# Keys and queries of an attention layer turned by VectorE in squares of 32 instead of by TensorE

## The chip, the cores and the metric

One core of one Trainium2 chip runs one fused kernel. The metric is the device time of one execution in microseconds. TensorE (PE) multiplies matrices and can turn a 128x128 tile by a product with the identity; VectorE (DVE), ScalarE (ACT) and GpSimd (POOL) work elementwise; SyncE (SP) issues all the DMAs, on one queue that 16 DMA engines serve.

## What is computed

Attention with 4 sink keys and a sliding window of 128, then two feed-forward layers on its output. In float32 throughout:

```python
scores = q @ k.T / sqrt(64)                  # q, k, v: (2, 8, 768, 64)
keep = is_sink | ((rel >= 0) & (rel < 128))  # 4 sinks, window of 128
a = softmax(where(keep, scores, -1e9))
x = (a @ v), heads side by side              # (1536, 512)
p = domain_probs / sum(domain_probs)
x = sum_e p[:, e] * (relu(x @ w1[e]) @ w2[e])     # 4 experts, 1024 wide
h = x @ w_in; out = (h * cos(h)) @ w_out          # 2048 wide
```

## The kernel before, in words

The 1536 tokens are T = 12 tiles of 128; tiles 0 to 5 are the first sequence, 6 to 11 the second. The attention runs in ROUNDS = 27 rounds, numbered i from 0; tile t has rounds 2t and 2t+1, with four heads in each. Every engine has its own list of instructions in program order, and semaphores tie the lists together. An engine that waits holds up all that is behind in its list.

In a round PE makes the scores of two pairs of heads (`scores`, L1406), turns the weights of the round before (`turn_weights`, L1417), turns the next keys in an odd round and the next queries in an even one (`turn_keys`, L1349, and `turn_queries`, L1368: four turns of 128x128 into `turn_bank`), and multiplies the weights of three rounds ago with the values (`weigh_values`, L1441; the sinks' part is L1455, the turn of the sinks' weights and sums L1382). Round i, odd, turns the keys of tile (i+3)/2; round i, even, the queries of tile i/2+1. The scores of a pair wait until the masks of the pair two before it are done, since they share two pairs of banks.

DVE merges and masks the scores (`merge`, L1042, `mask_head`, L1058), then copies the turned keys out of PSUM (`copy_keys`, L1069), in an odd round; the turned queries are copied by ACT (L796), but for tiles 7, 8 and 9 by DVE (`copy_queries`, L1075). It then does the sinks and the inverses of the sums (L1082 to L1099), and in some rounds sums of weights (L1121, rounds 8 and 10) or of tokens (L1129, rounds 18 to 23) for the first feed-forward block, and the low halves of its tokens (`tokens_lo`, L1136). ACT takes the exponentials (L779) and copies the turned weights out (L787). POOL cuts the turned weights to the window (`part_weights`, L595 and L598), and in every even round from 6 on it multiplies a tile of the output by its inverse sums (`normalise`, L651), which come back from memory by DMA (`store_inverse`, L428, and `load_norm`, L436).

SP issues in a written order. Keys (L410), queries (L416) and values (L422) of a tile are loads of 256 KB in pieces of 256 bytes, 1024 of them. After the weights w1 (L443), the values of tile 2 and the probabilities (L506), a loop over t issues `load_norm(t-3)`, `load_keys(t+3)`, `store_inverse(t-2)`, `load_queries(t+3)` and `load_values(t)`.

After round 24 PE goes over to the feed-forward blocks, which fill the rest of the time; their first products are put between the last rounds of attention.

## Time and profile before

| | |
|---|---|
| runs, median (lowest to highest) | 835.33 us (834.03 to 837.50) |
| profiled execution, whole | 837.64 us |
| its span | 835.9 us |
| PE busy | 831.0 us, 99% of the span |
| VectorE busy | 455.7 us, 55% |
| ScalarE busy | 458.0 us, 55% |
| GpSimd busy | 551.7 us, 66% |
| DMA queue of SP | 100976 packets, 69.58 MB, 28.5% of 16 engines |
| attention, from the first product to the last values | about 3 to 95 us |

The profile is one execution. Its page has busy times, the span cut into 40 slices, the DMA queues, and the chain of work that ended last. The trace behind it gives each instruction's start, and for an idle time what ended it. The granted clock is 1.00 in every stretch.

### The profile page before, as it was taken

To read this page: it belongs to the slowest core of one execution; us is meant where nothing else is said; L and a number is where in the kernel's file an instruction comes from. 1 tells how busy PE (TensorE), PEld (TensorE's weight loads), DVE (VectorE), ACT (ScalarE), POOL (GpSimd) and SP (SyncE) were. 2 spreads that over 40 slices of the span, in tenths; PEclk is the share of its full clock that TensorE was granted. 3 is DMA by queue.
4 is the path that set the end of the run, shared out by engine and by line. 5 is a ranking of instruction groups with operands and counts; after the bars stand their busy time and mean duration, and the time that the engine had idled before them with its cause. 6 is when DMAs were issued, how large, how long until landed. Compare 5 with 4: busy or idle time off the path is not lost.

```text
span 835.9 us, 13778 instructions
## 1 busy us (share of the span) xinstructions
PE 831.0 (99%) x4564; PEld 743.6 (89%) x4564; DVE 455.7 (55%) x947; ACT 458.0 (55%) x985; POOL 551.7 (66%) x417
## 2 busy tenths in 40 slices
PE   9999999999999999999999999999999999999998
PEld 7777989988988988988988998998998998998997
DVE  4988833523523427633433433338767749756756
ACT  5888734334334435433423523525867869867864
POOL 3777996476476778575475575878384399685450
PEclk9999999999999999999999999999999999999999
DMA  8785231211221220432331131130223430530202
GB/s 184 169 190 147 67 123 51 102 61 44 98 68 44 91 83 19 117 105 53 95 112 50 52 101 51 51 101 30 73 63 76 125 117 0 177 102 18 84 1 76
DMA packets 101045, 70.46 MB, mean 84 GB/s; under 512 B 68368, under 2 KB 74864, under 8 KB 100976
## 3 DMA queue, kind: packets, MB, share of 16 engines
q1 hardware_dynamic: 100976, 69.58, 28.5%
q8 instruction: 39, 0.64, 0.3%
q14 instruction: 30, 0.25, 0.1%
HBM read 62.96 MB, written 3.19 MB: 79 GB/s over the span
## 4 chain that ended last, share of the span: by engine, by line
PE 96%; DVE 1%; issue 1%; ACT 1%; DMA 0%; SPq 0%; ACTq 0%; DVEq 0%
PE scores L1499 11%; PE scores L1503 11%; PE scores L1501 11%; PE scores L1512 10%; PE scores L1514 10%; PE scores L1510 10%; PE bank L1512 5%; PE bank L1514 5%; PE bank L1510 5%; PE bank L1499 3%; PE bank L1501 3%; PE bank L1503 3%; PE scores L1406 2%; PE bank L1441 2%; PE bank L1417 1%
## 5 line engine op out<-in xcount | busy, mean ns | idle before, releaser
L665 POOL TENSOR_TENSOR w_lo<-w_raw,w_hi 128x512 fp32r<-128x512 f32 x96 | 129.8, 1362 | 139.0 <-ACT w_hi L814 139.0
L1499 PE MATMUL scores<-x_hi,w_hi 128*128 128x384 f32 x528 | 177.1, 335 | 0.4 <-DVE x_lo L1136 0.2
L1503 PE MATMUL scores<-x_hi,w_lo 128*128 128x384 f32 x528 | 176.8, 335 | 0.0
L1501 PE MATMUL scores<-x_lo,w_hi 128*128 128x384 f32 x528 | 176.5, 334 | 0.0
L672 POOL TENSOR_TENSOR w_lo<-w_raw,w_hi 128x1024 fp32r<-128x1024 f32 x48 | 116.2, 2431 | 65.4 <-ACT w_hi L824 65.4
L824 ACT ACTIVATE w_hi<-w_raw 128x1024 fp32r<-128x1024 f32 x48 | 50.9, 1060 | 190.2 <-PE scores L1514 188.8
L1514 PE MATMUL scores<-w_hi,h_lo 128*128 128x512 f32 x384 | 149.3, 389 | 0.0
L1512 PE MATMUL scores<-w_lo,h_hi 128*128 128x512 f32 x384 | 149.3, 389 | 0.0
L1510 PE MATMUL scores<-w_hi,h_hi 128*128 128x512 f32 x384 | 149.0, 388 | 0.0
L1240 DVE SCALAR_TENSOR_TENSOR acc<-scores,probs,acc 128x512 f32<-128x512 f32 x56 | 41.8, 749 | 116.5 <-PE scores L1514 116.5
L1499 PEld LDWEIGHTS scores<-x_hi,w_hi 128*128 128x128 f32 x528 | 99.1, 188 | 2.4 <-issue 0.7
L1501 PEld LDWEIGHTS scores<-x_lo,w_hi 128*128 128x128 f32 x528 | 99.1, 188 | 0.9
L1503 PEld LDWEIGHTS scores<-x_hi,w_lo 128*128 128x128 f32 x528 | 99.1, 188 | 0.0
L665 POOL TENSOR_TENSOR w_lo<-w_sum,w_hi 128x768 fp32r<-128x768 f32 x48 | 92.5, 1928 | 0.0
L1514 PEld LDWEIGHTS scores<-w_hi,h_lo 128*128 128x128 f32 x384 | 72.1, 188 | 14.9
L1510 PEld LDWEIGHTS scores<-w_hi,h_hi 128*128 128x128 f32 x384 | 72.1, 188 | 14.1
L1512 PEld LDWEIGHTS scores<-w_lo,h_hi 128*128 128x128 f32 x384 | 72.1, 188 | 14.0
L1512 PE MATMUL bank<-w_lo,h_hi 128*128 128x512 f32 (+1 forms) x196 | 76.0, 388 | 0.0
L1514 PE MATMUL bank<-w_hi,h_lo 128*128 128x512 f32 (+1 forms) x196 | 75.9, 387 | 0.0
L1510 PE MATMUL bank<-w_hi,h_hi 128*128 128x512 f32 (+1 forms) x196 | 75.8, 387 | 0.0
L660 POOL TENSOR_TENSOR w_sum<-w_raw 128x512 f32<-128x512 f32 x46 | 59.5, 1293 | 15.8 <-DMA w_raw<-in_moe_w_in_dram 13.6
L1204 DVE SCALAR_TENSOR_TENSOR h_lo<-scores,h_hi 128x384 fp32r<-128x384 f32 x64 | 35.5, 554 | 44.1 <-ACT h_hi L878 42.6
(140 smaller groups left out, 1548.0 us busy)
## 6 DMA issues: line engine op xcount, KB each, us to landing
w_raw<-in_moe_w_dram SPq DMA_DIRECT2D x30, 1024.0 KB, 5.1
w_raw<-in_moe_w_in_dram SPq DMA_DIRECT2D x8, 1024.0 KB, 5.0
w_raw<-in_moe_w_out_dram SPq DMA_DIRECT2D x8, 1024.0 KB, 5.4
v_nat<-in_v_dram SPq DMA_DIRECT2D x12, 256.0 KB, 4.0
norm<-routing_dram SPq DMA_DIRECT2D x24, 128.0 KB, 3.2
x_t<-t_sum SPq DMA_DIRECT2D x192, 16.0 KB, 1.9
k_nat<-in_k_dram SPq DMA_DIRECT2D x11, 256.0 KB, 3.8
q_nat<-in_q_dram SPq DMA_DIRECT2D x11, 256.0 KB, 3.6
```

The source lines that it names most:

```text
L660: nc.gpsimd.tensor_tensor(*weight_sum(n)).then_inc(w1_summed, 1)
L665: nc.gpsimd.tensor_tensor(w1_slots(w1_lo, h % 2, part), w1_part(h % 2, part), w1_slots(w1_hi, h % 2, part).bitcast(F32), ALU.subtract)\
L672: nc.gpsimd.tensor_tensor(w2_lo[:, i::2], w2_raw[:, i::2], w2_hi[:, i::2].bitcast(F32), ALU.subtract)\
L824: nc.scalar.activation(w2_hi[:, i::2], w2_raw[:, i::2], ACT.Copy).then_inc(w2_hi_ready, 1)
L1204: nc.vector.scalar_tensor_tensor(h_part(h_lo, h % 2, c), c_source(h % 2, c), 0.0, h_part(h_hi, h % 2, c).bitcast(F32), ALU.max, ALU.subtract)\
L1240: kept_one = nc.vector.scalar_tensor_tensor(acc[:, n], down_bank[k][:], probs[:, n, e:e + 1], acc[:, n], ALU.mult, ALU.add)
L1499: nc.tensor.matmul(target[:, 0:HALF], w1_hi[:, i, slot, d], x_hi[:, n - 1, d], start=first and d == 0, stop=False, skip_group_check=True)
L1501: nc.tensor.matmul(target[:, 0:HALF], w1_hi[:, i, slot, d], x_lo[:, n - 1, d], start=False, stop=False, skip_group_check=True)
L1503: last = nc.tensor.matmul(target[:, 0:HALF], w1_lo[:, i, slot, d], x_hi[:, n - 1, d], start=False, stop=d == 1, skip_group_check=True)
L1510: nc.tensor.matmul(target[:, cols], h_hi[:, i, f, toks], w2_hi[:, c, cols], start=i == 0 and f == 0, stop=False, skip_group_check=True)
L1512: nc.tensor.matmul(target[:, cols], h_hi[:, i, f, toks], w2_lo[:, c, cols], start=False, stop=False, skip_group_check=True)
L1514: return nc.tensor.matmul(target[:, cols], h_lo[:, i, f, toks], w2_hi[:, c, cols], start=False, stop=i == 1 and f == 1, skip_group_check=True)
```

## The change

The keys of the second sequence (tiles 6 to 11) and the queries of tiles 7, 8 and 9 no longer pass through PE. SP loads them in pieces of 32 elements (128 bytes), so that each square of 32x32 lands at the place where its turned form belongs, and one `nc.vector.transpose` of 128x512 turns the sixteen squares of a tile in place of the copy out of PSUM. The squares lie in memory that x_hi and x_lo take later. A key load has 24 pieces on each of 32 partitions (768), and there are 16; a query load has 12 on each (384), and there are 16. They are issued in turns t = 1 to 5 of SP's loop: 6, 6 and 4 of keys, then 8 and 8 of queries. `copy_keys` of tile 6 waits for all 16 key loads, the turn of the queries of tile 7 for all 16 of queries. The loads of keys 6 to 11 and of queries 7 to 9 by L410 and L416 go. In DVE's list `sum_tokens(3)` moves from round 23 to behind three `tokens_lo`.

```diff
-QUERIES_BY_DVE = (7, 8, 9)
+SQUARE_QUERIES = (7, 8, 9)
...
+    SQUARE_KEYS = TPB
...
+            def load_squares(dst, src, first, last, part, signal):
+
+                h = part // 2
+                p, r = divmod(h, 2)
+                for f in range(2):
+                    rows = slice((2 * r + f) * 32, (2 * r + f + 1) * 32)
+                    source = src[1, h, (first - TPB) * P:(last - TPB) * P, f * 32:(f + 1) * 32]
+                    sp.dma_start(dst[rows, p, :].rearrange("j (c i) -> j c i", i=32),
+                                 source.rearrange("(c j) i -> j c i", j=32)).then_inc(signal, 16)
...
-                if 5 <= t + 3 < T:
+                if 5 <= t + 3 < SQUARE_KEYS:
                     load_keys(t + 3)
                 if t >= 2:
                     store_inverse(t - 2)
-                if 5 <= t + 3 < T:
+                if 5 <= t + 3 < T and t + 3 not in SQUARE_QUERIES:
                     load_queries(t + 3)
                 if 3 <= t < T:
                     load_values(t)
+                if t in (1, 2, 3):
+                    for part in range(((0, 6, 12, 16)[t - 1]), (0, 6, 12, 16)[t], 2):
+                        load_key_squares(part)
+                elif t in (4, 5):
+                    for part in range(8 * (t - 4), 8 * (t - 3), 2):
+                        load_query_squares(part)
...
             def copy_keys(t):
-                dve.wait_ge(k_turned, t + 1)
+                if t < SQUARE_KEYS:
+                    dve.wait_ge(k_turned, t + 1)
+                else:
+                    dve.wait_ge(k_squares_landed, 16 * 16)
...
+                    n = t - SQUARE_KEYS
+                    nc.vector.transpose(target, k_squares[:, :, n * P:(n + 1) * P]).then_inc(k_ready, 1)
+
+            def turn_queries(t):
+
+                dve.wait_ge(q_squares_landed, 16 * 16)
                 dve.wait_ge(scores_done, PAIRS * (t - 1))
...
+                nc.vector.transpose(q_t[:, t % 2], q_squares[:, :, n * P:(n + 1) * P]).then_inc(q_squares_ready, 1)
...
-                if i in (18, 20, 21, 23):
-                    sum_tokens((18, 20, 21, 23).index(i))
-                if i == 22:
-                    tokens_lo(0, 0)
+                if i in (18, 20, 21):
+                    sum_tokens((18, 20, 21).index(i))
+                if i in (22, 23):
+                    tokens_lo(0, (22, 23).index(i))
                 if i == ND:
-                    tokens_lo(0, 1)
                     tokens_lo(0, 2)
+                    sum_tokens(3)
                     tokens_lo(0, 3)
                     tokens_lo(0, 4)
...
-                if i % 2 == 1 and (i + 3) // 2 < T:
+                if i % 2 == 1 and (i + 3) // 2 < SQUARE_KEYS:
                     turn_keys((i + 3) // 2)
-                elif i >= 2 and i % 2 == 0 and i // 2 + 1 < T:
+                elif i >= 2 and i % 2 == 0 and i // 2 + 1 < T and i // 2 + 1 not in SQUARE_QUERIES:
                     turn_queries(i // 2 + 1)
```

SP's list between the probabilities and the values of tile 4, before:

```order
L506 DMA probs_in<-in_moe_domain_probs_dram 128x12x4
L410 DMA k_nat<-in_k_dram 128x8x64
L428 DMA routing_dram<-inverse 8x128
L416 DMA q_nat<-in_q_dram 128x8x64
L436 DMA norm<-routing_dram 64x4x128 x2
L410 DMA k_nat<-in_k_dram 128x8x64
L428 DMA routing_dram<-inverse 8x128
L416 DMA q_nat<-in_q_dram 128x8x64
L422 DMA v_nat<-in_v_dram 128x8x64
L436 DMA norm<-routing_dram 64x4x128 x2
L410 DMA k_nat<-in_k_dram 128x8x64
```

and now, up to the values of tile 4 (the lines are those of the changed kernel):

```order
L543 DMA probs_in<-in_moe_domain_probs_dram 128x12x4
L445 DMA k_squares<-in_k_dram 32x24x32 x6
L428 DMA k_nat<-in_k_dram 128x8x64
L465 DMA routing_dram<-inverse 8x128
L435 DMA q_nat<-in_q_dram 128x8x64
L445 DMA k_squares<-in_k_dram 32x24x32 x6
L473 DMA norm<-routing_dram 64x4x128 x2
L465 DMA routing_dram<-inverse 8x128
L435 DMA q_nat<-in_q_dram 128x8x64
L459 DMA v_nat<-in_v_dram 128x8x64
L445 DMA k_squares<-in_k_dram 32x24x32 x4
L473 DMA norm<-routing_dram 64x4x128 x2
```

Six square loads stand ahead of the keys of tile 5, and twelve ahead of the first `norm`; the later loads of k_nat are gone.

PE's list in rounds 12 and 13, before:

```order
L1406 MATMUL scores<-k_t,q_t 128x128 x4
L1417 MATMUL bank<-ident,weights 128x128 x4
L1368 MATMUL bank<-ident,q_nat 128x128 x4
L1455 MATMUL bank<-sink_t,v_sink 128x128 x4
L1441 MATMUL bank<-weights_t,v_nat 64x128 x8
L1406 MATMUL scores<-k_t,q_t 128x128 x4
L1417 MATMUL bank<-ident,weights 128x128 x4
L1349 MATMUL bank<-ident,k_nat 128x128 x4
L1382 MATMUL bank<-ident,sink_w 104x128
L1441 MATMUL bank<-weights_t,v_nat 64x128 x8
```

and now:

```order
L1464 MATMUL scores<-k_t,q_t 128x128 x4
L1475 MATMUL bank<-ident,weights 128x128 x4
L1513 MATMUL bank<-sink_t,v_sink 128x128 x4
L1499 MATMUL bank<-weights_t,v_nat 64x128 x8
L1464 MATMUL scores<-k_t,q_t 128x128 x4
L1475 MATMUL bank<-ident,weights 128x128 x4
L1437 MATMUL bank<-ident,sink_w 104x128
L1499 MATMUL bank<-weights_t,v_nat 64x128 x8
```

Four turns are gone from each of the two rounds; nine rounds (9, 11 to 17 and 19) change in this way.

## Rows read from the trace of the kernel before

**Rows 1.** The page: busy PE, and the DMA share in 40 slices of the span

```profile
PE 831.0 (99%) x4564; PEld 743.6 (89%) x4564; DVE 455.7 (55%) x947; ACT 458.0 (55%) x985; POOL 551.7 (66%) x417
DMA  8785231211221220432331131130223430530202
```

**Rows 2.** Busy time by stretch: start:end, length, engines' busy us (instructions), clock, DMA share, GB/s

```profile
20.00:40.00 20.00, 19.95 (x201) 15.33 (x197) 17.78 (x82) 16.30 (x62) 14.24 (x26) 1.00 0.79 181
46.77:75.37 28.60, 28.60 (x290) 22.83 (x292) 23.54 (x113) 25.46 (x93) 21.32 (x35) 1.00 0.67 166
100.00:120.00 20.00, 20.00 (x95) 17.23 (x94) 7.76 (x13) 7.03 (x12) 19.77 (x15) 1.00 0.30 97
```

**Rows 3.** Chain of work that ended last, rounds 13 and 14: start, us, what

```profile
50.48 0.44 PE bank L1349 x4
50.92 0.11 PE bank L1382
...
53.73 0.44 PE bank L1368 x4
```

**Rows 4.** Timeline of round 7: start, us, engine, line, what

```profile
29.12 1.16 PE L1406 MATMUL scores<-k_t,q_t 64*128 64x264 f32 x8
29.89 0.43 DVE L1042 COPY_PREDICATED scores<-in_prev,scores 128x256 f32<-128x256 int32 x1
30.71 0.60 PE L1349 MATMUL bank<-ident,k_nat 128*128 128x128 f32 x4
32.37 0.94 PE L1406 MATMUL scores<-k_t,q_t 64*128 64x264 f32 x6
32.59 0.30 DVE L1099 COPY inverse<-bank 8x128 f32<-8x128 f32 x1
```

**Rows 5.** DVE's copies out of PSUM and turns of squares: ns min/median/max, first and last start

```profile
L1069 DVE COPY k_t<-bank x11: 687/687/691, 9.5 to 70.4; 128x512 f32<-128x512 f32 x11
L1075 DVE COPY q_t<-bank x3: 687/689/691, 47.9 to 60.9; 128x512 f32<-128x512 f32 x3
L1264 DVE STREAM_TRANSPOSE t_sum<-acc x12: 668/686/712, 338.3 to 648.2; 128x512 f32<-128x512 f32 x12
```

**Rows 6.** SP's issues on the timeline; the time is that of issuing

```profile
20.23 0.84 SPq L506 DMA_DIRECT2D probs_in<-in_moe_domain_probs_dram  x1
21.12 4.57 SPq L410 DMA_DIRECT2D k_nat<-in_k_dram  x1
...
28.39 1.35 SPq L436 DMA_DIRECT2D norm<-routing_dram  x2
```

**Rows 7.** The load of keys issued at 21.12 us: from issue to landing

```profile
DMA to landing us min/median/max: 7.1/7.1/7.1
```

**Rows 8.** DMA in 8 to 9.25 us (pieces of 256 bytes)

```profile
DMA packets 1346, 0.34 MB, mean 271 GB/s; under 512 B 1346, under 2 KB 1346, under 8 KB 1346
q1 hardware_dynamic: 1346, 0.34, 124.5%
```

**Rows 9.** DMA in 23.5 to 24 us (mostly the probabilities, pieces of 16 bytes)

```profile
DMA packets 939, 0.07 MB, mean 132 GB/s; under 512 B 933, under 2 KB 933, under 8 KB 937
```

**Rows 10.** DMA in 350 to 358 us (pieces of 128 bytes, sparse)

```profile
q1 hardware_dynamic: 1737, 0.20, 15.6%
```

**Rows 11.** Timeline of rounds 9 to 12, the places that wait for a load or for DVE

```profile
38.13 1.09 PE L1441 MATMUL bank<-weights_t,v_nat 128*64 128x128 f32 x16
38.57 0.69 DVE L1069 COPY k_t<-bank 128x512 f32<-128x512 f32 x1
...
43.75 0.42 DVE L1042 COPY_PREDICATED scores<-in_prev,scores 128x256 f32<-128x256 int32 x1
46.73 0.42 PEld L1417 LDWEIGHTS bank<-ident,weights 128*128 128x128 f32 x4 [0.27 <-ACT weights L779]
```

**Rows 12.** POOL's first product with a norm, and its wait

```profile
32.83 1.27 POOL L651 TENSOR_TENSOR x_t<-x_t,norm 128x512 f32<-128x512 f32 x1 [3.02 <-DMA norm<-routing_dram]
```

**Rows 13.** PE's first instruction of the second product of the feed-forward layer

```profile
87.31 0.44 PE L1499 MATMUL scores<-x_hi,w_hi 128*128 128x384 f32 x1 [0.20 <-DVE x_lo L1136]
```

More of the change, by code:

```diff
@@ L108, in sem @@
             return ctx.enter_context(nc.semaphore(name))
+        early = ExitStack()
+        sb("early_hi", [P, 2, 2, HALF], stack=early)
+        q_squares = sb("q_squares", [P, PAIRS, HALF], stack=early)
+        sb("early_lo", [P, 5, 2, HALF], stack=early)
+        k_squares = sb("k_squares", [P, PAIRS, S], stack=early)
+        early.close()
         x_hi = sb("x_hi", [P, 7, 2, HALF], F32R)
@@ L186, in program @@
         first_landed = [sem("first_keys_landed"), sem("first_queries_landed")]
+        k_squares_landed = sem("k_squares_landed")
+        q_squares_landed = sem("q_squares_landed")
         probs_landed = sem("probs_landed")
@@ L204, in program @@
         q_ready = sem("q_ready")
+        q_squares_ready = sem("q_squares_ready")
         k_sink_kept = sem("k_sink_kept")
@@ L291, in prev_at, with turned_by_pe @@
             return SLOT - own_at(t)
+        def turned_by_pe(t):
+            return sum(n not in SQUARE_QUERIES for n in range(t))
         def heads(src, t):
@@ L414, in load_queries, with load_key_squares, load_query_squares @@
                 if t >= 2:
-                    sp.wait_ge(q_turned, t - 1)
+                    before = max(n for n in range(t) if n % 2 == t % 2 and n not in SQUARE_QUERIES)
+                    sp.wait_ge(q_turned, turned_by_pe(before) + 1)
                 sp.dma_start(q_nat[:, t % 2, :].rearrange("p (h d) -> p h d", h=H), heads(q, t))\
                     .then_inc(q_landed[t % 2], 16)
+            def load_squares(dst, src, first, last, part, signal):
[6 more added lines that the diff above has]
+                                 source.rearrange("(c j) i -> j c i", j=32)).then_inc(signal, 16)
+            def load_key_squares(part):
+                load_squares(k_squares, k, SQUARE_KEYS, T, part, k_squares_landed)
+            def load_query_squares(part):
+                load_squares(q_squares, q, SQUARE_QUERIES[0], SQUARE_QUERIES[-1] + 1, part, q_squares_landed)
             def load_values(t):
@@ L791, in copy_queries @@
             def copy_queries(t):
-                act.wait_ge(q_turned, t + 1)
+                act.wait_ge(q_turned, turned_by_pe(t) + 1)
                 if t >= 2:
@@ L923, in _ @@
                     exp_head(i, 3)
-                if i >= 2 and i % 2 == 0 and i // 2 + 1 < T and i // 2 + 1 not in QUERIES_BY_DVE:
+                if i >= 2 and i % 2 == 0 and i // 2 + 1 < T and i // 2 + 1 not in SQUARE_QUERIES:
                     copy_queries(i // 2 + 1)
@@ L1068, in copy_keys @@
                     dve.wait_ge(k_sink_kept, (t - 3) // TPB + 1)
-                nc.vector.tensor_copy(k_t[:, :, t % 3, 0:P], turn_bank[:].rearrange("p (k s) -> p k s", k=PAIRS))\
-                    .then_inc(k_ready, 1)
-            def copy_queries(t):
-                dve.wait_ge(q_turned, t + 1)
+                target = k_t[:, :, t % 3, 0:P]
+                if t < SQUARE_KEYS:
+                    nc.vector.tensor_copy(target, turn_bank[:].rearrange("p (k s) -> p k s", k=PAIRS))\
+                        .then_inc(k_ready, 1)
+                else:
+                    n = t - SQUARE_KEYS
+                    nc.vector.transpose(target, k_squares[:, :, n * P:(n + 1) * P]).then_inc(k_ready, 1)
+            def turn_queries(t):
+                dve.wait_ge(q_squares_landed, 16 * 16)
                 dve.wait_ge(scores_done, PAIRS * (t - 1))
-                nc.vector.tensor_copy(q_t[:, t % 2], turn_bank[:].rearrange("p (k s) -> p k s", k=PAIRS))\
-                    .then_inc(q_ready, 1)
+                n = t - SQUARE_QUERIES[0]
+                nc.vector.transpose(q_t[:, t % 2], q_squares[:, :, n * P:(n + 1) * P]).then_inc(q_squares_ready, 1)
             def copy_sinks(t):
@@ L1152, in _ @@
                     copy_keys((i + 3) // 2)
-                elif i % 2 == 0 and i // 2 + 1 in QUERIES_BY_DVE:
-                    copy_queries(i // 2 + 1)
+                elif i % 2 == 0 and i // 2 + 1 in SQUARE_QUERIES:
+                    turn_queries(i // 2 + 1)
                 if i % 2 == 0 and 0 <= (i - 2) // 2 < T:
@@ L1360, in turn_queries @@
             def turn_queries(t):
-                pe.wait_ge(q_landed[t % 2], 16 * (t // 2 + 1))
+                pe.wait_ge(q_landed[t % 2], 16 * sum(n % 2 == t % 2 and n not in SQUARE_QUERIES for n in range(t + 1)))
                 if t == 1:
                     pe.wait_ge(first_ready, 2)
+                elif t < SQUARE_KEYS:
+                    pe.wait_ge(k_ready, t)
                 else:
-                    pe.wait_ge(k_ready, t)
+                    pe.wait_ge(q_ready, turned_by_pe(t) - 1)
                 target = out_bank if t == 1 else turn_bank
@@ L1390, in scores @@
                 else:
-                    pe.wait_ge(q_ready, t)
+                    if t in SQUARE_QUERIES:
+                        pe.wait_ge(q_squares_ready, SQUARE_QUERIES.index(t) + 1)
+                    else:
+                        pe.wait_ge(q_ready, turned_by_pe(t))
                     pe.wait_ge(k_ready, t)
```

## The prediction

> **What bounds the kernel now.** I read the page first: PE is busy 99% of the span, while the other three compute engines have a third or more of it free, and the DMA queue is near its full share only in the first slices [rows 1]. Then the stretches: PE has no idle time to speak of in attention, and none later, where DVE does 7.76 us of work in 20 [rows 2]. So a microsecond taken from PE's list in attention moves all that follows it, and so does each microsecond for which PE is made to wait there. DVE is close behind: 17.78 of 20 us in 20 to 40 us. So is the DMA queue, at a share of 0.79 in the same stretch [rows 2]. The change takes from the first and adds to the last, so the question is whether the loads come in time.
>
> **What goes from PE.** In the chain of work four turns of keys take 0.44 us of PE's time, and four turns of queries as much [rows 3]. Nine such steps go: 9 x 0.44 = 3.96 us. Two of them, in rounds 9 and 11, lie where PE waits for others: between round 10 and round 12 DVE carries the sums of weights, round 11's masks start only when those end, and PE's turn of weights in round 12 waits for ACT behind them [rows 11]. Removing PE's work ahead of that wait brings nothing. Seven are left: 7 x 0.44 = 3.1 us.
>
> **Whether DVE can follow.** From round 12's masks to round 21's PE has 28.6 us of work in 28.6 us and DVE 23.54 [rows 2]. Less 3.1, PE still has 25.5, so DVE is not the bound over the whole. It is in single rounds. An odd round such as 7 costs PE 3.25 us (29.12 to 32.37) and DVE 3.0 (29.89 to 32.89) [rows 4]. PE falls to 2.81, DVE stays, and in rounds 17 and 19, where work is dense on both, some 0.2 to 0.3 us each is not gained. I take 2.6 of the 3.1.
>
> **What DVE does instead.** Nine copies out of PSUM of 687 to 689 ns become nine turns of the same 128x512. The kernel already has this turn, out of SBUF: 668 to 712 ns, median 686 [rows 5]. So the exchange costs nothing either way: 9 x 0.03 us at the extremes, 0.2 us up or down. PSUM is left alone and k_t is written as before.
>
> **The move at the end.** Before, PE's second product waits 0.20 us for a `tokens_lo` of DVE that stands behind `sum_tokens(3)` [rows 13]. With the sum moved back that wait goes, a gain of 0.2 us at most 0.3. The sum feeds the last of the seven products, some microseconds later, so its delay is hidden by the products before it.
>
> **What the DMA queue gets.** Key squares: 16 x 768 = 12288 pieces of 128 bytes, query squares 16 x 384 = 6144; the nine loads that go had 9216 of 256 bytes. The bytes are the same, the pieces double, and they come all at once, from 21 to some 45 us. The price of a piece is the open term. Three rows bound it. Pieces of 256 bytes in a full queue: 1346 in 1.25 us, 0.93 ns a piece for the 16 engines together [rows 8]. Pieces of 16 bytes: 939 in 0.5 us, 0.53 ns [rows 9]. Pieces of 128 bytes, but between places on chip and thinly spread: 15.6% of 16 engines for 8 us over 1737 pieces, 11.5 ns of one engine, 0.72 ns for the 16 together [rows 10]. I take 0.72, the row of this size and also the middle of the others. Above 0.93 lies one more bound: counted as engine time, the 256-byte piece takes 124.5% x 16 x 1250 / 1346 = 18.5 ns, or 1.16 ns a piece if pieces stop overlapping [rows 8].
>
> **When the loads come.** Before, SP is held for 4.57 us while it issues the keys of tile 5, to 25.7 us, since the weights and the probabilities are still in the queue; they land at 21.12 + 7.1 = 28.2 us [rows 6, 7]. That is 1.55 us after their own 0.95 us of pieces. Now six square loads (4608 pieces, 3.3 us) stand ahead of them: 31.5 us. PE wants them at 30.71 [rows 4], so it waits 0.8 us.
>
> All key squares: from 25.7 on the queue has 12288 x 0.72 = 8.8 us of squares, four ordinary loads (keys 5, queries 5 and 6, values 3) of 0.95 = 3.8, and the first norm, 256 KB at 271 GB/s = 1.0. That ends at 39.4 and lands at 40.9. DVE wants them for tile 6 in round 9, where it now starts the copy at 38.57 [rows 11]. It stands in the list until 40.9: **2.3 us late** (the 0.8 is inside this). Queued behind it are the sinks, the masks of round 10 and the sums of weights, which leave no idle time, so PE in round 12 is 2.3 us late too.
>
> Beside it: values 3 land at 38.7, PE wants them at 38.13 + 0.8, in time. The first norm lands at 36.8, 4.0 us late. POOL waits for it already (3.02 us, to 32.83) and has the cutting of weights for PE's round 9 behind it [rows 12], about 2.5 us after that start, so 39.3 where PE would come at 38.9: 0.4 us, hidden under the 2.3. Query squares: two norms, two loads of values and 6144 pieces more, 1.0 + 0.95 + 2.2 twice, end at 47.7 and land at 49.3; DVE wants them at 47.9 + 2.3 = 50.2 [rows 5]. In time, with 0.9 us to spare.
>
> **The sum.** + 2.3 (late squares) - 2.6 (turns) - 0.2 (end) = -0.5 us. The span of 835.9 becomes 835.4. The profiled execution took 837.64 in all, 2.3 us more than the median of the runs; I set the change against the median: 835.33 - 0.5 = **834.8 us**.
>
> **Rivals.**
>
> A, the squares come in time. At 0.53 ns a piece the keys of tile 5 land at 30.6 and all key squares at 38.5, just when they are wanted. Then nothing is late: -2.6 - 0.2 = -2.8, **832.5 us**. For it: the 16-byte row. Against: a square is eight times as long. The Trainium skill ("DMA: Bandwidth & Descriptors", section "Why small descriptors are slow (HBM only)") gives a packet a fixed 3 cycles beside one for each 32 bytes; 256 bytes are 11 cycles and 128 are 7. By that rule, as an estimate, the piece costs 0.59 ns, near this rival. The trace agrees only in part: 16-byte pieces should then be four times cheaper than 256-byte ones, and are less than two times.
>
> B, the squares are as dear as whole pieces, and the wait for them replaces the turns. At 1.16 ns the keys of tile 5 land at 33.5, all key squares at 47.2 (8.7 late), the query squares at 58.9 where DVE wants them at 56.6: 11 us late, less 2.8: +8.2, **843.5 us**. It turns slower by over 0.5% once DVE is 7 us late, from about 1.06 ns a piece. For it: the source is memory, read by half rows, and each load writes only 32 partitions. Against: the engines did overlap pieces in every full stretch.
>
> B', the same at 0.93 ns: 4.9 us late for the keys, 5.3 for the queries, +2.5: **837.8 us**, no measurable change.
>
> C, all nine turns count, and the loads are in time: -3.96 - 0.2, **831.1 us**. It needs rounds 9 to 11 to be less tied to DVE than rows 11 say.
>
> D, that PE's turns don't go. The order shows four fewer in each of nine rounds; no chance of its own.
>
> **Chances.** Forecast 0.33, A 0.24, B' 0.19, C 0.10, B 0.14. 0.5% is 4.2 us, about what a measurement of this kernel can tell from no change. Faster by more: only C, 0.10. Slower by more: B, 0.14. Within: 0.76. The range goes from C, 831.0, to a little above B', 838.5, and leaves out B.
>
> **What would show it.** PE's matmuls fall by 36, and rounds 13 to 16 are 0.44 us shorter each. The key load for tile 5 lands near 31.5 us, and PE waits up to 1 us in round 7. DVE's first turn of k_squares has an idle time ahead of it that ends by DMA at about 41 us; idle there under 0.5 us is A, over 5 is B. The turn takes 0.69 us. The wait of PE's second product is gone. What would make all of it wrong: SP held at another point of its list, so that a norm or a load of values comes later than the squares do, or one engine of the 16 with a longer queue than the others, since a load lands with its last.

## The result, and the profile after the change

The kernel before took 834.68 us in these runs (median, 833.92 to 837.5), the changed one **843.7 us** (840.91 to 845.98): a ratio of 1.0099, with a 95% interval of 1.0071 to 1.0127. The change makes the kernel 9 us slower. The forecast was 834.8 us and a range up to 838.5. The mean granted clock of TensorE was 0.992 to 0.998 in the six runs of the changed kernel, and 1.00 in every run of the kernel before that was timed beside the experiments.

The page of the changed kernel, its profiled execution 845.23 us: busy time of the engines, then the granted clock of TensorE and the DMA share in 40 slices. They answer to [rows 1].

```profile
span 843.5 us, 13720 instructions
PE 829.8 (98%) x4528; PEld 740.4 (88%) x4528; DVE 457.1 (54%) x947; ACT 458.2 (54%) x985; POOL 551.8 (65%) x417
PEclk9889999999999999999999999999999999999999
DMA  9864233311311311323421221220323430530202
```

The turns have gone: 4528 matmuls for 4564. But PE's clock is down in slices 2 and 3. The stretches of the same trace say where (columns as in [rows 2]: busy us of PE, PEld, DVE, ACT, POOL; clock; DMA share; GB/s):

```profile
20.00:40.00 20.00, 16.71 (x142) 12.71 (x140) 13.39 (x57) 11.75 (x43) 7.72 (x14) 0.83 0.88 167
40.00:60.00 20.00, 14.90 (x147) 11.45 (x147) 13.35 (x61) 13.29 (x50) 16.23 (x27) 0.92 0.67 138
30.50:36.00 5.50, 5.42 (x30) 3.87 (x31) 2.10 (x9) 0.15 (x1) 0.00 (x0) 0.50 0.97 180
57.00:64.00 7.00, 6.84 (x45) 5.33 (x47) 4.68 (x25) 4.90 (x19) 4.45 (x4) 0.53 0.48 117
```

From 20 to 40 us PE starts 142 matmuls; before it was 201 [rows 2]. Some of that is idle time, and some is work at a granted clock of 0.50 and 0.53, which is the lower of the two levels, 1.2 GHz in place of 2.4. PE's timeline of the changed kernel gives the single waits (in brackets: idle us before the instruction, and who ended it):

```profile
30.58 1.11 PE L1401 MATMUL bank<-ident,k_nat 128*128 128x128 f32 x4 [3.29 <-DMA k_nat<-in_k_dram]
...
31.84 1.98 PE L1499 MATMUL bank<-weights_t,v_nat 128*64 128x128 f32 x16
33.75 2.13 PE L1464 MATMUL scores<-k_t,q_t 64*128 64x264 f32 x8
...
41.37 0.29 PE L1437 MATMUL bank<-ident,sink_w 128*104 128x128 f32 x1 [1.18 <-POOL sink_w L655]
41.59 1.09 PE L1499 MATMUL bank<-weights_t,v_nat 128*64 128x128 f32 x16
...
57.16 0.43 PE L1437 MATMUL bank<-ident,sink_w 128*104 128x128 f32 x1 [3.40 <-DVE sink_w L1143]
57.51 1.98 PE L1499 MATMUL bank<-weights_t,v_nat 128*64 128x128 f32 x16
```

Three waits: 3.29 us for the keys of tile 5 in round 7, 1.18 us for POOL in round 9, 3.40 us for DVE in round 13. After the two long ones the same sixteen products of values take 1.98 us, after the short one 1.09. The first of the three is not the same in every execution: in other runs that issue the same six square loads ahead of the keys of tile 5, PE waited 1.34 us (`half_pieces`), 1.70 (`keys_only`) and 1.01 (`norm_first`) there, with the clock full behind it. What came later made up for that: in round 11 PE's scores start at 46.62 and 47.41 us in the first two, at 46.15 in the changed kernel.

Behind them stand the loads. SP's timeline shows what its issues took, DVE's and POOL's show who waits for what lands:

```profile
20.40 5.57 SPq L445 DMA_DIRECT2D k_squares<-in_k_dram  x6
26.01 1.89 SPq L428 DMA_DIRECT2D k_nat<-in_k_dram  x1
...
28.91 4.18 SPq L445 DMA_DIRECT2D k_squares<-in_k_dram  x6
33.13 1.35 SPq L473 DMA_DIRECT2D norm<-routing_dram  x2
...
36.14 3.85 SPq L445 DMA_DIRECT2D k_squares<-in_k_dram  x4
...
42.31 5.06 SPq L445 DMA_DIRECT2D q_squares<-in_q_dram  x8
...
49.79 4.16 SPq L445 DMA_DIRECT2D q_squares<-in_q_dram  x8
```

```profile
41.85 0.71 DVE L1121 STREAM_TRANSPOSE k_t<-k_squares 128x512 f32<-128x512 f32 x1 [0.58 <-DMA k_squares<-in_k_dram]
...
55.68 0.71 DVE L1128 STREAM_TRANSPOSE q_t<-q_squares 128x512 f32<-128x512 f32 x1 [4.38 <-DMA q_squares<-in_q_dram]
```

```profile
37.32 1.61 POOL L694 TENSOR_TENSOR x_t<-x_t,norm 128x512 f32<-128x512 f32 x1 [11.08 <-DMA norm<-routing_dram]
```

The 32 square loads take SP 22.8 us of issuing (5.57 + 4.18 + 3.85 + 5.06 + 4.16) in the 33.6 us from 20.4 to 54.0, and the ordinary loads between them fill the rest: SP has under 1 us free there. In the later part, where the queries are issued, the 16 DMA engines are not full (a share of 0.67 from 40 to 60 us, against 0.97 from 30.5 to 36), so it is SP that holds the query squares back. Each of their loads is there soon after it is issued:

```profile
L445 SPq DMA_DIRECT2D q_squares<-in_q_dram x16: 456/470/1192, 42.3 to 53.5; - x16
...
DMA to landing us min/median/max: 2.0/2.3/3.0
```

(The first row has the time of one issue in ns, lowest, median and highest, the second the time from issue to landing.) The keys of tile 5 are issued at 26.0 in place of 21.1 [rows 6]. The first norm, for which POOL waited 3.02 us before [rows 12], now leaves POOL idle for 11.08. And DVE waits 4.38 us for the query squares, with the sums of round 13 behind that turn in its list.

### The profile page after: what moved, and what is told of

It is laid out like the page before. It is cut to its first block, busy times and chain, and to the rows that moved or that the text cites. A ratio compares the mean times of both kernels' runs of the same rounds, so it can differ in the third digit from the quotient of the medians.

```text
span 843.5 us, 13720 instructions
## 1 busy us (share of the span) xinstructions
PE 829.8 (98%) x4528; PEld 740.4 (88%) x4528; DVE 457.1 (54%) x947; ACT 458.2 (54%) x985; POOL 551.8 (65%) x417
## 4 chain that ended last, share of the span: by engine, by line
PE 92%; SPq 4%; issue 1%; DMA 1%; DVE 1%; ACT 1%; POOL 0%; ACTq 0%; DVEq 0%; POOLq 0%
PE scores L1557 11%; PE scores L1561 11%; PE scores L1559 11%; PE scores L1572 10%; PE scores L1570 10%; PE scores L1568 10%; PE bank L1570 5%; PE bank L1572 5%; PE bank L1568 5%; PE bank L1557 3%; PE bank L1559 3%; PE bank L1561 3%; SPq L445 2%; PE bank L1499 1%; PE scores L1464 1%
```

## The experiments

All ratios are to the kernel before, timed on the same chip; its medians were 834.1 to 834.8 us. The code cuts show the main lines of each edit; `...` marks what is left out, and a name on the right says which run the lines belong to.

**Each half alone.** `keys_only` leaves the queries as they were before. `queries_only` does the reverse: the key squares go, and PE turns all keys.

```
-SQUARE_QUERIES = (7, 8, 9)            keys_only
+SQUARE_QUERIES = ()
+QUERIES_BY_DVE = (7, 8, 9)
...
-    SQUARE_KEYS = TPB                 queries_only
+    SQUARE_KEYS = T
...
```

> The changed kernel with its key squares alone: the queries of tiles 7 to 9 are turned by PE and copied by DVE as before, and the 16 loads of query squares are gone. Theory (late loads, and PE at half its clock after a long wait): PE's wait of 3.3 us for the keys of tile 5 in round 7 and the slow stretch behind it stay (some 6 us), the wait for query squares (4.4 us on DVE) and the slow stretch behind that go; six turns of keys are saved. About 839 us. Rival (the squares cost by their turns on DVE, wherever the loads stand): six of nine turns are left, so about two thirds of the loss, 841 us, with PE's busy stretches as in the changed kernel.

> The changed kernel with its query squares alone: the keys of all tiles go by PE as before, and the 16 loads of key squares are gone. Theory (late loads): nothing stands ahead of the keys of tile 5, so PE doesn't wait in round 7; the 16 query loads come in turns 4 and 5 of SP's loop and should land at about 47 us, just when DVE wants them, so 834 us, with at most 2 us of wait. Rival (the squares cost by their turns on DVE): three of nine turns, a third of the loss, 838 us.

Keys alone: 839.31 us, 1.0057 (1.0035 to 1.0079). Queries alone: 836.31 us, 1.0024 (1.0011 to 1.0036). Both halves cost time, and 5.0 + 2.0 us is less than the 9 us of both. The first is the time that the theory gave, though by another path: PE waits 1.70 us in round 7, not 3.3, and its long wait is for POOL. The second lies between the theory's 834 and the rival's 838. In `keys_only`:

```profile
29.03 0.66 PE L1398 MATMUL bank<-ident,k_nat 128*128 128x128 f32 x4 [1.70 <-DMA k_nat<-in_k_dram]
...
40.34 0.43 PE L1434 MATMUL bank<-ident,sink_w 128*104 128x128 f32 x1 [4.30 <-POOL sink_w L653]
```

In `queries_only` PE waits for nothing over 0.6 us before the query squares; DVE waits 2.99 us for them, though nothing but the ordinary loads stood ahead of them. So the query half is late by itself, and not only because the keys held the queue.

**What is left when nothing has to be loaded.** `no_loads` issues no square at all; DVE and ACT fill the squares once with zeros, and DVE turns these. The second sequence's keys and three of its queries are then zero.

```
-                if t in (1, 2, 3):
-                    for part in range(((0, 6, 12, 16)[t - 1]), (0, 6, 12, 16)[t], 2):
-                        load_key_squares(part)
-                elif t in (4, 5):
-                    for part in range(8 * (t - 4), 8 * (t - 3), 2):
-                        load_query_squares(part)
...
+            nc.vector.memset(k_squares[:], 0.0).then_inc(k_squares_landed, 1)
```

> The changed kernel without any load of squares: their memory is set once at the start, by DVE and ACT, while both wait for the first scores. This leaves out the keys of tiles 6 to 11 and the queries of tiles 7 to 9, so the attention of the second sequence isn't computed from them; the lists of PE and DVE stay as changed. It is what the nine saved turns are worth when no load is in the way. Theory (DVE is the next bound): rounds 12 to 23 gain 1.8 us, as they do with the plain loads of the run before, so 832.3 us. The forecast's own figure was 2.8 to 3.1, so 831.5. Rival (the lists themselves are slower): 834 or more.

831.97 us, 0.9966 (0.9951 to 0.9981): 2.4 us below the kernel before on the same chip (834.4), and by the interval 1.6 to 4.1. The forecast had 2.6 + 0.2. In PE's timeline the removed turns give less: `no_loads` is 0.60 us ahead of `reorder_only` (below) in round 9, before any turn is gone (scores at 31.91 for 32.51), and 2.23 in round 20 (65.29 for 67.52), so 1.6 us came in the rounds between. It is also the best case, since the nine ordinary loads are gone too and nothing stands in their place. The exchange of engines gains 1.6 to 2.4 us; the whole loss, 843.7 - 832.0 = 11.7 us, belongs to the loads.

**Few long loads.** `cheap_loads` fetches the same bytes in 8 loads of 128 partitions with one contiguous stretch for each partition; the values in the squares are then in the wrong places. Half of the keys' bytes, in place of six sixteenths, are now issued ahead of the keys of tile 5.

```
-                load_squares(k_squares, k, SQUARE_KEYS, T, part, k_squares_landed)
+                flat = k[1].rearrange("h s d -> (h s d)").rearrange("(p n) -> p n", p=P)
+                sp.dma_start(k_squares[:, part // 4, :], flat[:, part // 4 * S:(part // 4 + 1) * S])
...
-                    for part in range(((0, 6, 12, 16)[t - 1]), (0, 6, 12, 16)[t], 2):
+                    for part in range(((0, 8, 12, 16)[t - 1]), (0, 8, 12, 16)[t], 4):
...
```

> The changed kernel, but the squares' memory is filled by four plain loads of keys (pieces of 3 KB) and four of queries (1.5 KB) at the same turns of SP's loop, the same bytes. This leaves out that each square lands in its place, so the keys and queries of the second sequence aren't the right ones; every instruction of PE and DVE stays. Theory (late loads): no wait for keys or squares, the nine turns saved count as forecast, 832 us (a fall of 2 to 3 from before). Rival (turns on DVE, or PE and DVE no longer fitting together): 841 to 844 us, as the changed kernel.

834.54 us, 1.0005 (0.9993 to 1.0017). Neither expectation holds exactly: the 9 us go, but 2.6 us of what `no_loads` shows do not come back. POOL still waits 6.51 us for the first norm and PE 1.58 us for POOL. So the bytes, brought forward to where the queue is full, use up the gain even in eight long loads.

**Many loads, few pieces.** `whole_pieces` keeps all 32 loads at their places and of their sizes, but lets each read one contiguous stretch for each partition (again with values in the wrong places): 32 pieces a load in place of 768 and 384.

```
-                    source = src[1, h, (first - TPB) * P:(last - TPB) * P, f * 32:(f + 1) * 32]
+                    n = (last - first) * P
+                    source = src[1].rearrange("h s d -> (h s d)").rearrange("(p n) -> p n", p=P)[rows, p * n:(p + 1) * n]
```

> The changed kernel with its 32 square loads at the same places, each to the same 32 partitions and of the same bytes, but of one contiguous stretch of 3 KB (queries: 1.5 KB) for each partition, so 32 pieces a load in place of 768 and 384. The values in the squares are then in the wrong places, and the output isn't the reference's; all else is the same. Theory (a load costs its issue, whatever is in it): SP needs 0.45 to 0.5 us for each of the 32, PE waits for the keys of tile 5, POOL for the norm and DVE for the query squares as in the changed kernel: 842 to 844 us. Rival (the pieces cost): the waits go, as with eight long loads: 834 to 835 us. Between them, 837 to 839 us, the full queue's part comes from the pieces (issues of the first six loads under 0.6 us) and the rest from the issues.

837.6 us, 1.0041 (1.0026 to 1.0055): the case between, though its sign (the first six issues under 0.6 us each) did not come; they took 0.81, and it is the later groups of keys that became short. SP's timeline of this run, against the same lines of the changed kernel above:

```profile
19.81 4.87 SPq L446 DMA_DIRECT2D k_squares<-in_k_dram  x6
24.72 0.42 SPq L428 DMA_DIRECT2D k_nat<-in_k_dram  x1
...
26.16 2.90 SPq L446 DMA_DIRECT2D k_squares<-in_k_dram  x6
...
32.58 2.49 SPq L446 DMA_DIRECT2D k_squares<-in_k_dram  x4
...
37.40 5.03 SPq L446 DMA_DIRECT2D q_squares<-in_q_dram  x8
...
44.84 3.81 SPq L446 DMA_DIRECT2D q_squares<-in_q_dram  x8
```

The key loads fall from 13.60 to 10.26 us of issuing (five other runs with small pieces, six loads of them ahead of the keys of tile 5, have 12.5 to 14.4), and the squares come at 38.25 us in place of 41.85. The query loads hardly fall: 8.84 us for 9.22, though their pieces are a twelfth. That is 0.55 to 0.58 us for each of the 16, whatever is in it.

**Half the pieces of the queries.** `half_pieces` loads only the first half of each query square's tokens; the other half is zero.

```
-  source = src[1, h, (first - TPB) * P:(last - TPB) * P, f * 32:(f + 1) * 32]
+  source = src[1, h, (first - TPB) * P:(first - TPB) * P + (last - first) * P // keep, f * 32:(f + 1) * 32]
...
```

> The changed kernel with the same 16 loads of query squares, each of half the pieces (192 in place of 384); the other half of that memory is set once at the start. This leaves out half of the queries of tiles 7 to 9. Theory (a load costs its issue, some 0.47 us of SP, and the pieces are hidden under it): the query squares land no earlier, DVE's wait of 4.4 us stays, 843 us. Rival (a load costs its pieces, the forecast's way of counting): they land 3 to 4 us earlier, the wait falls below 1.5 us, and with it the slow clock behind it goes: 838 us.

842.47 us, 1.0080 (1.0055 to 1.0104): the theory's side in time. Half the bytes and pieces of the queries bring 1.2 us by the medians, less than the two intervals tell apart; the two groups of eight take SP 5.50 and 3.97 us, 0.59 us a load. In its trace the query squares do come 2.2 us earlier and DVE waits 2.17 us for them, not 4.4:

```profile
40.34 5.50 SPq L446 DMA_DIRECT2D q_squares<-in_q_dram  x8
```

```profile
53.52 0.71 DVE L1129 STREAM_TRANSPOSE q_t<-q_squares 128x512 f32<-128x512 f32 x1 [2.17 <-DMA q_squares<-in_q_dram]
```

But SP began these loads 2.0 us earlier (40.34 for 42.31) because of what stood before them, which the edit leaves alone. From the first of them to the turn it is 13.2 us here, 13.4 in the changed kernel and 12.8 in `whole_pieces`: with 192, 384 or 32 pieces in a load the time is nearly the same.

Four runs make a ladder of medians: no loads 832.0, 8 long loads 834.5, 32 loads of long pieces 837.6, the changed kernel 843.7. Bytes (in eight loads) 2.6 us, 32 loads in place of 8 3.1, small pieces (and what follows from them, the lower clock too) 6.1. The steps are known only roughly: taken by the ratios to the kernel before they are 3.3, 3.0 and 4.8 us. And the middle one has two changes in it, since the 8 loads write 128 partitions each and the 32 write 32 each; no run parts the two.

**The order of the loads.** `five_first` issues the keys of tile 5 ahead of the first squares. `norm_first` puts a step between the groups, so that the first norm goes ahead of ten of the sixteen key squares.

```
-                if 5 <= t + 3 < SQUARE_KEYS:  five_first
-                    load_keys(t + 3)
+                if t == 1:
+                    load_keys(5)
...
-                if t in (1, 2, 3):            norm_first
+                if t in (1, 3, 4):
...
-                elif t in (4, 5):
+                elif t in (5, 6):
```

> The changed kernel with the keys of tile 5 loaded ahead of the first six loads of key squares; nothing else moves. Theory (order in the queue): PE's wait in round 7 (3.3 us) and the half clock behind it go, but the squares land as late as before, so DVE's waits for key squares and query squares come out longer by what was won; half of the gain is left, about 840.5 us. Rival (the order doesn't matter, since the squares are the last to land whatever stands first): 843.7 us.

> The changed kernel with the square loads of the second, third and later groups each issued one step later, behind the first norm: six key squares in step 1, six in step 3, four in step 4, query squares in steps 5 and 6. Theory (the first norm is what holds POOL, and with it PE in round 9): POOL's longest wait for a norm falls from 11.1 us to 5 to 7, and PE's wait of 1.2 us for POOL's sink weights in round 9 goes. In exchange DVE waits longer for the key squares in round 9, 4 to 6 us in place of 0.6, and PE's loss moves there: 843 to 845 us, no gain in time. Rival (POOL is held by the keys of tile 5 and by PE, not by the norm): its wait stays over 9 us and the time goes up by what DVE waits more, 846 to 849 us.

`five_first`: 842.32 us, 1.0084 (1.0061 to 1.0107), between theory and rival, and the interval takes in the changed kernel's ratio. The wait for the keys of tile 5 is gone, but PE waits 2.38 us for the queries of tile 6 behind them and 3.57 for POOL. `norm_first`: 849.75 us, 1.0188 (1.0174 to 1.0202), outside both expectations. POOL's wait for the first norm does fall, to 6.24 us, as the theory had it, but PE's wait for POOL in round 9 stays (1.33 us). DVE's rows show what the new order cost:

```profile
43.79 0.71 DVE L1122 STREAM_TRANSPOSE k_t<-k_squares 128x512 f32<-128x512 f32 x1 [5.73 <-DMA k_squares<-in_k_dram]
...
61.60 0.71 DVE L1129 STREAM_TRANSPOSE q_t<-q_squares 128x512 f32<-128x512 f32 x1 [8.21 <-DMA q_squares<-in_q_dram]
```

I had counted the first of these waits and not the second, which was 4.38 us in the changed kernel. Whichever load goes first, another is late: of the three orders the best is 1.4 us below the changed kernel, which the runs can't tell from nothing.

**Fewer tiles, later.** `four_tiles` turns only the keys of the last four tiles on DVE; its 16 loads are issued four at a time in steps 3 to 6, the queries are turned by PE.

```
-    SQUARE_KEYS = TPB
+    SQUARE_KEYS = 8
-                if t in (1, 2, 3):
+                if t in (3, 4, 5, 6):
+                    at = (3, 4, 5, 6).index(t)
+                    for part in range((0, 4, 8, 12, 16)[at], (0, 4, 8, 12, 16)[at + 1], 2):
```

> Only the keys of the last four tiles come as squares (16 loads of 512 pieces, four of them in each of the steps 3 to 6); the keys of tiles 5 to 7 and all queries are turned by PE. Theory (the loss is in loads that stand ahead of the keys of tile 5 and of the first norm, and PE's turns are worth what was removed): both come as before the change, four turns of 0.44 us go, about 0.3 us each counts: 833 to 833.5 us, 1 us below before. Rival (16 small loads cost SP 8 us of issue wherever they stand, and delay later norms and values): POOL waits over 6 us for a norm after 40 us and the time is 836 us or more.

840.97 us, 1.0080 (1.0066 to 1.0093): the rival's side in time, and by a mechanism near the one it names, though no wait of POOL for a norm is over 6 us. In round 11 PE is 0.6 us behind `reorder_only` (below; scores at 39.94 for 39.30), in round 14 it is 3.5 (51.95 for 48.44), with POOL waiting 2.57 us for a norm, and then the last group is late:

```profile
51.09 3.78 SPq L446 DMA_DIRECT2D k_squares<-in_k_dram  x4
```

```profile
56.70 0.71 DVE L1120 STREAM_TRANSPOSE k_t<-k_squares 128x512 f32<-128x512 f32 x1 [7.95 <-DMA k_squares<-in_k_dram]
```

Four loads with the norm, keys, store, queries and values of a step hold SP for 7.2 us (the groups start at 30.91, 38.14 and 45.39), and the two rounds of a step take PE 6.8 us (32.51 to 39.30 in `reorder_only`). SP itself is the bound there. No version that loads real squares beats the kernel before.

**The lower clock.** `filled` and `filled_less` put products that nobody reads ahead of PE's two long waits, 24 and 26 of them, then 12 and 13 (the trace counts each of them twice). The cut is that of `filled_less`.

```
+                if t == 5:
+                    pe.wait_ge(q_ready, t - 1)
+                    fill(turn_bank[:, 0:P // 2], 12)
...
+                if t == 5:
+                    fill(turn_bank[:, 0:P // 2], 13)
```

> The changed kernel with idle products (128x64, of zeros, into a bank that is free then) put where PE waits: 24 ahead of the turn of the keys of tile 5 and 26 ahead of the turn of the sinks of tile 5. The waits for loads stay. Theory A (PE's granted clock falls to half in a long wait and the work after it pays for that): the stretches 30.5 to 36 and 57 to 64 us run at full clock, 2.5 to 3 us are won at each, about 838 us. Theory B (the waits alone are the loss): 843.7 us or more. If the products outlast the waits they cost what is over.

> The changed kernel with products that nobody reads put in front of its two waits of over 3 us, as in the run with 24 and 26 fills, but 12 and 13 of them, since one fill took 0.22 to 0.23 us there. They should take 2.7 and 3.0 us and end just before the keys of tile 5 and the sinks come, so that PE is late by nothing new. Theory (half of the clock costs time by itself): the values and scores of round 7 take 1.1 us each in place of 2.0, and the same in round 14; the changed kernel ran 5.5 us and 7 us at a granted clock of about 0.5, 2.5 to 3 us lost each, part of it beside waits for other engines: 839 to 841 us. Rival (the time lost at half clock is hidden by the waits that follow, for DVE and POOL): 843 to 845 us, and PE's waits in rounds 9 and 14 grow by what its products gain.

`filled`: 844.9 us, 1.0116 (1.0087 to 1.0144), and it says little, since I had mis-sized the fills: they took 5.47 and 5.92 us and ended after the loads had come. `filled_less`: 841.69 us, 1.0101 (1.0085 to 1.0118). Its median is 2.0 us below that of the changed kernel, but its ratio to the kernel before is no lower (1.0101 for 1.0099), so the times don't show that anything was won. PE's rows show where the clock was kept and what came of it:

```profile
27.23 2.79 PE L1617 MATMUL bank<-t_sum 128*128 128x64 f32 x24
30.34 0.66 PE L1404 MATMUL bank<-ident,k_nat 128*128 128x128 f32 x4 [0.32 <-DMA k_nat<-in_k_dram]
...
31.04 1.09 PE L1504 MATMUL bank<-weights_t,v_nat 128*64 128x128 f32 x16
...
39.76 0.43 PE L1442 MATMUL bank<-ident,sink_w 128*104 128x128 f32 x1 [2.41 <-POOL sink_w L655]
40.12 1.98 PE L1504 MATMUL bank<-weights_t,v_nat 128*64 128x128 f32 x16
...
57.47 0.32 PE L1442 MATMUL bank<-ident,sink_w 128*104 128x128 f32 x1 [1.27 <-DVE sink_w L1143]
57.72 1.09 PE L1504 MATMUL bank<-weights_t,v_nat 128*64 128x128 f32 x16
```

With PE kept at work, the values take 1.09 us in both places. In round 9 this kernel is 2.8 us ahead of the changed one (scores at 35.60 for 38.44), but of that only 0.6 is left in round 10 (42.02 for 42.61) and nothing in round 11 (46.09 for 46.15): the wait for POOL grew from 1.18 to 2.41 us, and the lower clock now comes behind that. The second place pays in this pair: 0.7 us ahead in round 14 (58.74 for 59.42), 2.6 in round 15 (61.86 for 64.41), and it stays. `five_first` bears it out without any filling: its query squares are turned at 55.80 us, as late as in the changed kernel, its clock is full behind PE's wait, and in round 15 it is 3.2 us ahead (61.24). So the first stretch at the lower clock is hidden, as the rival said, and the second costs an execution that has it some 2.6 to 3.2 us. How much of the 9 us between the medians that is, the runs leave open.

**The order of the sums at the end.** `reorder_only` is the kernel before with this one edit. It also serves above and below as a second profile of the kernel before, whose instructions are the same up to round 22.

```
-                if i in (18, 20, 21, 23):
-                    sum_tokens((18, 20, 21, 23).index(i))
+                if i in (18, 20, 21):
+                    sum_tokens((18, 20, 21).index(i))
-                if i == 22:
-                    tokens_lo(0, 0)
+                if i in (22, 23):
+                    tokens_lo(0, (22, 23).index(i))
                 if i == ND:
-                    tokens_lo(0, 1)
                     tokens_lo(0, 2)
+                    sum_tokens(3)
```

> The kernel before with the one change in DVE's list at the end: the fourth sum of tokens behind three low halves. The forecast gives it 0.2 us; 834.1 us, which can't be told from no change. Rival: it costs, since the last product's block comes later, up to 1 us more.

834.31 us, 0.9996 (0.9984 to 1.0009): no change that can be measured. Its profile turned out to matter more than its time. The same lines in PE's timeline, first of the profiled execution before the change, then of `reorder_only`:

```profile
8.43 1.06 PE L1349 MATMUL bank<-ident,k_nat 128*128 128x128 f32 x4
...
12.66 1.06 PE L1349 MATMUL bank<-ident,k_nat 128*128 128x128 f32 x4
13.65 1.27 PE L1406 MATMUL scores<-k_t,q_t 64*128 64x264 f32 x8
```

```profile
7.38 0.60 PE L1349 MATMUL bank<-ident,k_nat 128*128 128x128 f32 x4
...
9.66 0.60 PE L1349 MATMUL bank<-ident,k_nat 128*128 128x128 f32 x4
10.37 1.16 PE L1406 MATMUL scores<-k_t,q_t 64*128 64x264 f32 x8
...
27.31 0.60 PE L1349 MATMUL bank<-ident,k_nat 128*128 128x128 f32 x4
```

The profiled execution on which the forecast rests did its first rounds with turns of 1.06 us in place of 0.60. It was 3.3 us late at the third round (13.65 for 10.37), and 3.4 us late when it took the keys of tile 5 (30.71 [rows 4] for 27.31). Its 837.64 us stand 3.4 us above the 834.21 of this run: the whole difference lay in the opening. It was no single case: four of the 23 runs of the kernel before that were timed beside this one took 837.5 to 837.8 us, the others 833.7 to 835.7. And not only PE was late in it. SP was done issuing the keys of tile 5 at 25.7 us and they landed at 28.2 [rows 6, 7]; in `reorder_only` it was done at 22.1 (19.84 + 2.27), and they landed 5.0 us after 19.84, at 24.8.

## Why the prediction was wrong, point by point

**What goes from PE, whether DVE can follow, the move at the end: right in kind.** There are 36 matmuls fewer, and the turns are worth 1.6 to 2.4 us for the 2.6 of the forecast. In `no_loads` rounds 13, 14 and 15 are 0.34 to 0.43 us shorter than in `reorder_only`, near the 0.44 that I gave as a sign; but rounds 16 and 17 gain only 0.14 each, and rounds 9 and 12 become 0.22 and 0.50 us longer by waits for POOL and ACT. The turn took 705 to 714 ns, 0.02 us above the copies of [rows 5], inside the 0.2 us that I allowed for nine. The move at the end brought nothing that can be measured; 0.2 had been forecast, which such runs can't tell from it.

**The price of the square loads: the step that failed.** I priced the 32 loads by their pieces on the 16 DMA engines, 18432 x 0.72 ns = 13.3 us, and gave SP's issuing no time of its own. SP took 22.8 us for them. For the queries it was 9.2 us where I had 2.2 twice, and `half_pieces` and `whole_pieces` show that the pieces hardly enter there: it is 0.55 to 0.59 us a load. (No run issues the squares from a second engine's list, which would test SP's part directly.) For the keys, where a load has 768 pieces and the queue is full, pieces did count: they make up 3.3 of the 13.6 us of issuing. So the query squares, which were to land at 49.3 us with 0.9 to spare, were turned at 55.68, after a wait of 4.38.

**When the loads are wanted and when they come: two errors that cancelled.** I took these times from a profiled execution 2.3 us above the median, saw that, and wrote it off against the end of the span. Its surplus lay ahead of all these loads. In `reorder_only` PE wants the keys of tile 5 at 27.3 us and not at 30.71, DVE the squares of keys at 35.4 and not at 38.57 and the queries at 44.3 and not at 47.9, POOL the first norm at 26.4 and not at 29.8 (29.62 less its wait of 3.20). Against these times the changed kernel's squares were 6.5 us late for the keys (41.85) and 11.4 for the queries.

It looks as if the supply had been forecast well: keys of tile 5 at 31.5, measured 30.6; key squares 40.9, measured 41.85; norm 36.8, measured 37.3. That was luck. The supply started from the same late execution, from SP done at 25.7 us, where it was done at 22.1 in `reorder_only` and at 23.2 and 23.7 in `queries_only` and `four_tiles`, which have no squares ahead of that load either. From there my price puts all key squares at 37.3 to 38.9 us; they were turned 1.5 to 4.9 us after that in the six kernels that issue all 16 loads in small pieces by t = 3 (40.4 to 42.2). With both times from a usual execution the forecast's working gives a lateness of 1.9 to 3.5 us in place of 2.3, so 834.3 + 1.9 - 2.8 = 833.4 us to 834.3 + 3.5 - 2.8 = 835.0, about the forecast. The odd execution hid the error in the price, and did not make it.

**The POOL path.** "0.4 us, hidden" for the norm became a wait of PE of 1.18 us in the changed kernel and of 4.30 in `keys_only`. Part of that is the late norm, part a reading: from the product with the norm to PE's turn of the sinks' weights it takes not 2.5 us but 3.24 (37.10 to 40.34 in `keys_only`). That PE's wait for POOL grows when PE comes earlier (`filled_less`) shows that norm, keys and squares are three late loads side by side: the latest counts, and the removal of one uncovers the next.

**The clock.** The lower clock after PE's waits was not in the forecast at all. In the profiled execution it costs up to some 3 us, behind the second long wait.

**Where the profiled execution lost its time.** Set against `reorder_only`, PE in the changed kernel is 6.9 us late at the scores of round 10 (42.61 for 35.76), still 6.7 in round 13 (52.34 for 45.63), 12.4 in round 15 (64.41 for 51.97), and then regains 1.4 us, to 11.0 at the end of the span. So there are two losses, one up to round 10 behind the keys of tile 5, the norm and the key squares, and one in rounds 13 and 14 behind the query squares and the clock. The second is smaller where the clock stays full: `five_first` goes from 8.1 us late in round 11 (47.37 for 39.30) to 9.3 in round 15.

**The rivals.** B gave 843.5 us, nearly the measured time, from 11 us of lateness at the query squares, and 11.4 were measured. That is half luck: B's 1.16 ns a piece is not what made them late, since pieces hardly enter for the queries, and it had 8.7 us at the key squares, where 6.5 were measured. Nor did my sign tell the rivals apart. I had written that an idle time of DVE under 0.5 us ahead of the first turn of squares is A and over 5 is B; it was 0.58, because DVE was held up by PE's own waits, while the squares were 6.5 us late. B' (837.8 us) priced pieces alone as well. I had named the danger ("SP held at another point of its list") as what would make all of it wrong, without a price. It could have been priced: [rows 6] has 0.7 us for each norm's issue, and 32 issues of some 0.6 us are 19 us of SP in the 26.6 that the forecast had for all that is issued from 21.1 to 47.7 us, where the ordinary loads took another 9.9.

A's trace would have shown no long wait, and nothing speaks for it; C, with all nine turns counting and no load late, is 831.1 us, and even `no_loads` had 831.97. The rule of the Trainium skill named beside A ("DMA: Bandwidth & Descriptors", section "Why small descriptors are slow (HBM only)") doesn't decide the case: with 32 pieces a load, `whole_pieces` is still 3 us slower than before. And I worked it out wrongly for the 16-byte pieces: as an estimate by that rule they would be about three times cheaper than 256-byte ones (3.5 to 4 cycles for 11), not four. The row behind 0.53 ns is a mixture besides, 0.07 MB in 939 pieces, 70 bytes on average. For B, the loss reaches 7 us at about 1.0 ns a piece and not at 1.06, if the queries are counted as B counts them.

## What to carry to other kernels

Before times are read from one profiled execution, set it against the median, and find where the difference lies: what lies ahead of the place in question moves the times when a load is wanted and the times when it comes, and both must be taken from the same, usual execution. A load that is cut up has three prices, its bytes, its pieces and its issue; for the loads of 48 KB here the issue was the one that counted, so count the issues and the time that the issuing engine has in a stretch before counting descriptors. And where PE is busy throughout, taking 2 us from its list is worth less than one wait of 3 us, which costs itself and in part of the runs the lower clock behind it.

## What the runs showed of the hardware

- PE's granted clock fell to the lower level after waits of 3.29 and 3.40 us (above), 4.30 (`keys_only`), 3.57 (`five_first`), 3.39 (`half_pieces`) and 2.41 (`filled_less`), and the products behind it were at full speed after 1.18, 1.27, 2.38 and 2.36 (`five_first`) and 2.60 (`whole_pieces`). After 1.85 us in `filled` it fell. The 1.85 and the 2.60, each with the products of values behind it:

```profile
41.30 0.29 PE L1442 MATMUL bank<-ident,sink_w 128*104 128x128 f32 x1 [1.85 <-POOL sink_w L655]
41.52 1.87 PE L1504 MATMUL bank<-weights_t,v_nat 128*64 128x128 f32 x16
```

```profile
37.46 0.29 PE L1437 MATMUL bank<-ident,sink_w 128*104 128x128 f32 x1 [2.60 <-POOL sink_w L655]
37.68 1.09 PE L1499 MATMUL bank<-weights_t,v_nat 128*64 128x128 f32 x16
```

  The length of a wait alone does not say which it will be.
- In the opening of the profiled execution before the change the clock column shows 1.00 while turns take 1.06 us, near the 1.11 that they have at the lower level (at 30.58 us in the changed kernel). Whether the clock was low there isn't shown; the column alone does not show that such an opening is slow, the durations do.
- A query-square load of 384, 192 or 32 pieces holds SP 0.58, 0.59 and 0.55 us on average, a key-square load 0.85 us with 768 pieces and 0.64 with 32. An ordinary load of queries, with 1024 pieces, holds it 0.38 to 0.41 us when the queue has room.
